# Attention and two MLP layers on one core: k and v in one buffer, constants in paired transfers, one row correction moved to GpSimd

## The reference, cut to what matters

```python
kv  = einsum('bhsd,bhse->bhde', k, v)          # linear attention
out = einsum('bhsd,bhde->bhse', q, kv)
x   = out / sqrt(mean(out*out, -1) + 1e-6) * g_norm
u   = x + real(fft(fft(x, axis=1), axis=2))    # over tokens, then over features
y   = u + relu(layer_norm(u) @ w_ch1) @ w_ch2  # first MLP
z   = y + (U, V mix of tokens)                 # rank 32
out = z + relu(z @ w2_ch1) @ w2_ch2            # second MLP
```

## Time and profile before

| what | value |
|---|---|
| median of the runs | 1747.55 us |
| the profiled execution | 1749.69 us |
| its span in the profile | 1747.9 us |
| mean granted TensorE clock | 0.995 of full |
| TensorE matmul busy | 1695.9 us (97%) |
| VectorE busy | 1377.2 us (79%) |
| GpSimd busy | 223.1 us (13%) |
| bytes moved by DMA | 478.15 MB, 274 GB/s in the mean |

### The profile page before, as it was taken

The page is one execution under the profiler, slowest core; times in us unless marked ns, Lnnn a source line. Parts: engine busy times, 40 slices in busy tenths (PEclk is TensorE's granted clock), DMA queues, the critical chain, the costliest instruction groups (busy, mean ns, idle before and its releaser), DMA issues.

```text
span 1747.9 us, 27408 instructions
## 1 busy us (share of the span) xinstructions
PE 1695.9 (97%) x10712; PEld 1643.6 (94%) x10712; DVE 1377.2 (79%) x1741; ACT 802.0 (46%) x1163; POOL 223.1 (13%) x170
## 2 busy tenths in 40 slices
PE   5999989899999999999999999999999999999999
PEld 5888779899999999999999999999999999999999
DVE  5999989988887987986976867957857758659567
ACT  2344646545445445445444445434434444343343
POOL 0464320020020020020110110100100100100200
PEclk9999999999999999999999999999999999999999
DMA  8785569998988898898986777966867767767663
GB/s 252 253 278 193 212 240 363 382 343 303 328 312 307 325 318 303 321 323 306 317 284 241 287 235 267 335 226 243 281 220 251 267 237 253 265 223 252 226 249 122
DMA packets 118753, 478.15 MB, mean 274 GB/s; under 512 B 12897, under 2 KB 40865, under 8 KB 77922
## 3 DMA queue, kind: packets, MB, share of 16 engines
q1 hardware_dynamic: 118258, 475.22, 77.1%
q10 hardware_dynamic: 368, 1.18, 0.2%
HBM read 396.14 MB, written 78.64 MB: 272 GB/s over the span
## 4 chain that ended last, share of the span: by engine, by line
PE 77%; DVE 16%; issue 4%; DMA 3%; ACT 1%; SPq 0%; DVEq 0%; ACTq 0%
PE pair L977 11%; PE pair L978 11%; PE pair L979 11%; PE pair L1008 6%; PE pair L1009 6%; PE pair L1010 6%; PE pair L997 5%; PE pair L1000 5%; PE pair L999 5%; DVE t_lo L1628 4%; DMA sseq_sb<-s_seq 2%; PE pair L750 2%; DVE t_raw L1647 2%; PE pair L771 2%; PE tr_ps L865 1%
## 5 line engine op out<-in xcount | busy, mean ns | idle before, releaser
L977 PE MATMUL pair<-t_hi,w_sb 128*128 128x384 f32 x1344 | 461.6, 343 | 9.1 <-DVE h_sb L1665 7.2
L978 PE MATMUL pair<-t_lo,w_sb 128*128 128x384 f32 x1344 | 456.1, 339 | 0.0
L979 PE MATMUL pair<-t_hi,w_sb 128*128 128x384 f32 x1344 | 455.8, 339 | 0.0
L1295 ACT ACTIVATE t_hi<-t_raw 128x768 fp32r<-128x768 f32 x240 | 203.1, 847 | 280.0 <-DVE t_raw L1647 279.9
L1628 DVE TENSOR_TENSOR t_lo<-t_raw,t_hi 128x768 fp32r<-128x768 f32 x300 | 303.1, 1016 | 16.0 <-ACT t_hi L1283 14.6
L1874 POOL TENSOR_TENSOR t_raw<-a_sb 128x768 f32<-128x768 f32 x60 | 135.7, 2265 | 1277.5 <-PE pair L1000 553.6
L997 PE MATMUL pair<-w_sb,t_hi 128*128 128x256 f32 x1008 | 285.5, 283 | 8.7 <-DVE t_lo L1628 7.8
L999 PE MATMUL pair<-w_sb,t_hi 128*128 128x256 f32 x1008 | 282.7, 280 | 0.0
L1000 PE MATMUL pair<-w_sb,t_lo 128*128 128x256 f32 x1008 | 282.6, 280 | 0.0
L977 PEld LDWEIGHTS pair<-t_hi,w_sb 128*128 128x128 f32 x1344 | 253.3, 188 | 17.3 <-issue 12.7
L978 PEld LDWEIGHTS pair<-t_lo,w_sb 128*128 128x128 f32 x1344 | 253.2, 188 | 2.6
(11 more groups left out here) (189 smaller groups left out, 2196.3 us busy)
## 6 DMA issues: line engine op xcount, KB each, us to landing
w_sb<-wc SPq DMA_DIRECT2D x263, 1024.0 KB, 5.6
wc<-w_sb SPq DMA_DIRECT2D x25, 1024.0 KB, 6.6
w_raw<-wr1a SPq DMA_DIRECT2D x24, 512.0 KB, 7.6
w_raw<-wr1b SPq DMA_DIRECT2D x24, 512.0 KB, 4.1
w_raw<-wr2a SPq DMA_DIRECT2D x10, 1024.0 KB, 8.1
wc<-pb_v SPq DMA_DIRECT2D x16, 640.0 KB, 6.8
q_sb<-q_t SPq DMA_DIRECT2D x8, 1152.0 KB, 9.1
u_dram<-x_sb SPq DMA_DIRECT2D x24, 384.0 KB, 4.7
```

Of the source, the lines that this page charges most:

```text
L977: nc.tensor.matmul(ps, w_hi, hi[:, x, :], start=(fresh and x == 0), stop=False, skip_group_check=True)
L978: nc.tensor.matmul(ps, w_hi, lo[:, x, :], start=False, stop=False, skip_group_check=True)
L979: last = nc.tensor.matmul(ps, w_lo, hi[:, x, :], start=False, stop=(x == 1), skip_group_check=True)
L1295: nc.scalar.activation(t_hi[r][:, :, :], t_raw[r][:, :, :], ACT.Copy).then_inc(hi_ready, 1)
```

## The change

1. k and v stand in one buffer `in_kv`, [128, 5, 2, 512], and in one host tensor, and so each batch's `load_kv` is two transfers (1024 + 1024 KB in one, 128 + 128 KB in one) in place of four. Batch 0 comes in five pieces, one for each group of rows t, and each has its own semaphore: t = 0, 2 and the rest on SP, t = 1 and 3 on ScalarE's queue.
2. `cseq_sb` and `sseq_sb` become halves of one tensor `cs_sb`, [97, 2, 3, 289], loaded by one transfer; the sine half is padded from 96 to 97 rows. `cft_sb` and `sft_sb` become halves of `cf_sb`, [128, 2, 2, 257], also one transfer.
3. `fix_row(6)` goes from VectorE to GpSimd, between `add_transform(6, 1)` and `raw(0, 0)`; `add_transform(6, 2)` goes behind `raw(0, 0)`.
4. `copy_cos` of ScalarE waits for `ds_ready` of the batch before in place of `u_added`, and for `row_fixed` at tile 0 alone.

```diff
-    cseq_sb = at("cseq_sb", a0 + 38944, [PT + 1, NT, KC])
-    sseq_sb = at("sseq_sb", a0 + 42432, [PT, NT, KC])
+    cs_sb = at("cs_sb", a0 + 38944, [PT + 1, 2, NT, KC])
+    cseq_sb, sseq_sb = cs_sb[:, 0, :, :], cs_sb[0:PT, 1, :, :]
...
-                sp.dma_start(flat(k_sb[r][:, 0:4, :]), flat(k_main[b])).then_inc(kv_loaded[r], 16)
-                sp.dma_start(k_sb[r][0:64, 4, :], k_rest[b]).then_inc(kv_loaded[r], 16)
-                sp.dma_start(flat(v_sb[r][:, 0:4, :]), flat(v_main[b])).then_inc(kv_loaded[r], 16)
-                sp.dma_start(v_sb[r][0:64, 4, :], v_rest[b]).then_inc(kv_loaded[r], 16)
+                sp.dma_start(in_kv[r][:, 0:4, :, :].rearrange("p t x n -> p (t x n)"),
+                             kv_main[b].rearrange("p t x n -> p (t x n)")).then_inc(kv_loaded[r], 16)
+                sp.dma_start(flat(in_kv[r][0:64, 4, :, :]), flat(kv_rest[b])).then_inc(kv_loaded[r], 16)
...
-            for t in range(2):
-                sp.dma_start(flat(k_sb[0][:, 2 * t:2 * t + 2, :]), flat(k_main[0][:, 2 * t:2 * t + 2, :])).then_inc(kv0_loaded[t], 16)
-            sp.dma_start(k_sb[0][0:64, 4, :], k_rest[0]).then_inc(kv0_loaded[2], 16)
+            for t in (0, 2):
+                sp.dma_start(flat(in_kv[0][:, t, :, :]), flat(kv_main[0][:, t, :, :])).then_inc(kv0_loaded[t], 16)
+            sp.dma_start(flat(in_kv[0][0:64, 4, :, :]), flat(kv_rest[0])).then_inc(kv0_loaded[4], 16)
...
-            sp.dma_start(flat(cseq_sb[:, :, :]), flat(c_seq)).then_inc(const_loaded, 16)
-            sp.dma_start(flat(sseq_sb[:, :, :]), flat(s_seq)).then_inc(const_loaded, 16)
+            sp.dma_start(cs_sb[:, :, :, :].rearrange("p x t n -> p (x t n)"),
+                         cs_seq.rearrange("p x t n -> p (x t n)")).then_inc(const_loaded, 16)
             load_kv(2)
-            sp.dma_start(flat(cft_sb[:, :, :]), flat(c_feat)).then_inc(feat_loaded, 16)
-            sp.dma_start(flat(sft_sb[:, :, :]), flat(s_feat)).then_inc(feat_loaded, 16)
+            sp.dma_start(cf_sb[:, :, :, :].rearrange("p x t n -> p (x t n)"),
+                         cs_feat.rearrange("p x t n -> p (x t n)")).then_inc(feat_loaded, 16)
...
                 if not first:
-                    act.wait_ge(u_added, NT * (b - 1) + t + 1)
-                    act.wait_ge(row_fixed, b)
+                    act.wait_ge(ds_ready, NT * (b - 1) + t + 1)
+                    if t == 0:
+                        act.wait_ge(row_fixed, b)
...
                     unfold(b - 1, 2, first)
                     sum_slot(1)
-                    fix_row(b - 1)
...
-                for t in range(NT):
+                for t in range(NT if b < B - 1 else 2):
                     add_transform(b - 1, t)
+            fix_row(B - 2)
             raw(0, 0)
+            add_transform(B - 2, 2)
             raw(0, 2)
             raw(0, 3)
```

More of the change, by code:

```diff
@@ L175, in in_load_at, with build_program @@
     return t, t + 2
-def build_program(nc, k_main, k_rest, v_main, v_rest, q_t, g_norm, wr1a, wr2a, wr1b, wr2b, u_perm, v_perm,
-                  c_seq, s_seq, c_feat, s_feat, eye, u_dram, x2_dram, wc1, wc2, out):
+def build_program(nc, kv_main, kv_rest, q_t, g_norm, wr1a, wr2a, wr1b, wr2b, u_perm, v_perm,
+                  cs_seq, cs_feat, eye, u_dram, x2_dram, wc1, wc2, out):
     F32 = mybir.dt.float32
@@ L195, in build_program @@
     sets = (base + 31744, base)
-    k_sb = [at(f"k_sb{r}", sets[r], [128, 5, D]) for r in range(2)]
-    v_sb = [at(f"v_sb{r}", sets[r] + 10240, [128, 5, D]) for r in range(2)]
+    in_kv = [at(f"in_kv{r}", sets[r], [128, 5, 2, D]) for r in range(2)]
     q_sb = [at(f"q_sb{r}", sets[r] + 20480, [128, NP, 2 * NT * PT]) for r in range(2)]
@@ L216, in build_program @@
     ds_sb = at("ds_sb", a0 + 57760, [PT, NT, 2, LC])
-    cft_sb = at("cft_sb", a0 + 63936, [128, 2, LC])
-    sft_sb = at("sft_sb", a0 + 66016, [128, 2, LC])
+    cf_sb = at("cf_sb", a0 + 63936, [128, 2, 2, LC])
+    cft_sb, sft_sb = cf_sb[:, 0, :, :], cf_sb[:, 1, :, :]
     gn_sb = at("gn_sb", a0 + 68096, [PT, HD])
@@ L347, in build_program @@
         gn_loaded = sem("gn_loaded")
-        kv0_loaded, q0_loaded = [sem(f"kv0_loaded{n}") for n in range(3)], sem("q0_loaded")
+        kv0_loaded, q0_loaded = [sem(f"kv0_loaded{n}") for n in range(5)], sem("q0_loaded")
         kv_loaded, q_loaded = [[sem(f"{what}_loaded_{r}") for r in range(2)] for what in ("kv", "q")]
@@ L737, in first_kv_products @@
                         cols = slice(128 * h, 128 * (h + 1))
-                        last = nc.tensor.matmul(kv_ps[:, cols], k_sb[0][0:rows, t, cols], v_sb[0][0:rows, t, cols],
+                        last = nc.tensor.matmul(kv_ps[:, cols], in_kv[0][0:rows, t, 0, cols], in_kv[0][0:rows, t, 1, cols],
                                                 start=(t == 0 and h == 0), stop=(t == 4), skip_group_check=True)
@@ L749, in kv_products @@
                         rows = 128 if t < 4 else 64
-                        last = nc.tensor.matmul(kv_ps[:, cols], k_sb[r][0:rows, t, cols], v_sb[r][0:rows, t, cols],
+                        last = nc.tensor.matmul(kv_ps[:, cols], in_kv[r][0:rows, t, 0, cols], in_kv[r][0:rows, t, 1, cols],
                                                 start=(t == 0), stop=(t == 4))
@@ L1226, in phase1_step @@
                         ln_total(q)
-            for t in range(2):
-                act.dma_start(flat(v_sb[0][:, 2 * t:2 * t + 2, :]), flat(v_main[0][:, 2 * t:2 * t + 2, :])).then_inc(kv0_loaded[t], 16)
-            act.dma_start(v_sb[0][0:64, 4, :], v_rest[0]).then_inc(kv0_loaded[2], 16)
+            for t in (1, 3):
+                act.dma_start(flat(in_kv[0][:, t, :, :]), flat(kv_main[0][:, t, :, :])).then_inc(kv0_loaded[t], 16)
             act.wait_ge(warm_zeroed, 1)
@@ L1845, in add_transform, with fix_row @@
                 last.then_inc(u_added, 1)
+            def fix_row(b):
+                pool.wait_ge(u_added, NT * b + 1)
+                pool.wait_ge(mrow_ready, b + 1)
+                mirr = x_sb[b % 3][0:1, 1, :]
+                nc.gpsimd.tensor_tensor(mirr[:, 0:LC], mrow_sb[:, b % 2, 0:LC], nyq_sb[:, :], ALU.add)
+                nc.gpsimd.tensor_tensor(mirr[:, LC:D], mrow_sb[:, b % 2, LC:D], nyq_sb[:, 255:0:-1],
+                                        ALU.add).then_inc(row_fixed, 1)
             def sum_unit(unit):
@@ L1922, in transform_constants @@
     s_feat = np.sin(2 * np.pi * (((i[:, None] + 1) * l) % D) / D)
-    both = [a.reshape(2, 128, LC).transpose(1, 0, 2) for a in (c_feat, s_feat)]
-    return [np.ascontiguousarray(a, dtype=np.float32) for a in (c_seq, np.sin(angle), *both)]
+    s_seq = np.zeros((PT + 1, NT, KC))
+    s_seq[:PT] = np.sin(angle)
+    feat = np.stack([c_feat, s_feat]).reshape(2, 2, 128, LC).transpose(2, 0, 1, 3)
+    return [np.ascontiguousarray(a, dtype=np.float32) for a in (np.stack([c_seq, s_seq], axis=1), feat)]
 def kernel(q, k, v, g_norm, moe_w_ch1, moe_w_ch2, moe2_U, moe2_V, moe2_w_ch1, moe2_w_ch2):
@@ L1949 @@
     q_t = np.asarray(q)[:, :, order, :].reshape(B, NP, 2, PT, 2 * NT, HD).transpose(0, 2, 5, 1, 4, 3)
-    (k_main, k_rest), (v_main, v_rest) = rows(k), rows(v)
-    c_seq, s_seq, c_feat, s_feat = transform_constants()
+    kv = np.stack([rows(k), rows(v)], axis=2)
+    cs_seq, cs_feat = transform_constants()
     ins = {
-        "k_main": k_main, "k_rest": k_rest, "v_main": v_main, "v_rest": v_rest,
+        "kv_main": kv[:, :512].reshape(B, 128, 4, 2, D), "kv_rest": kv[:, 512:],
         "q_t": q_t.reshape(B, 128, NP, 2 * NT * PT), "g_norm": np.asarray(g_norm),
```

13 lines of the change are left out of this document (6 added, 7 removed).

## The result

The changed kernel takes **1757.5 us** in the median of five runs (1755.56 to 1759.53), against 1747.55 for the kernel before, run beside it (five runs, 1745.23 to 1752.44). The ratio is 1.0055, with a 95% interval of 1.0043 to 1.0067: slower by 0.55%. The profiled execution took 1757.5 us, its span 1755.7 us, 7.8 more than the span before, at a mean granted clock of 0.989 (before 0.995).

A forecast was written before the change was run, and what follows sets the result against it. TensorE, busy 97% of the span, was taken as the bound, so only its waits count: constants +10.3, seam -4.9, sum +5.4 us on the median 1747.55, giving 1753.0 us; 8-in-10 range 1748 to 1761.

The forecast's parts named there:

- +10.3 predicted: At the start, the paired constants land 10.3 us later, near 54.2 us, and TensorE starts its first transform there.
- the 24.7 that I took over: Time in us from which the prediction had the 97 cosine rows going through one DMA engine in the kernel before.
- a longer idle time costs no more than a few tenths: TensorE's half clock after its wait for the constants: a few tenths of a us more at most, left out.
- The rival that the constants land no later: At the start, constants land before 45.3 us; seam and up to 0.7 us remain, 1742; chance 0.07 with other faster ways.
- Edit 1 at nothing: The k and v loads: any saving ends under the wait for the constants, so priced at nothing.
- worth up to about 0.7 us: Start, were the constants on time: the fold's end at 43.30 and VectorE's chain would decide, worth up to about 0.7 us.
- 4.9 predicted: Seam at 217 to 230 us: step 6 starts at 239.1 in place of about 244.0, a gain of 4.9 us.
- I count one GpSimd instruction of delay each time: At the seam, VectorE's two-input instructions each wait for one GpSimd instruction; `lo_up(0, 0)` ends near 221.4 us.
- The rival of the held VectorE: VectorE held behind GpSimd's whole run at the seam: it gives 1.9 us, 1756; inside the forecast's chance of 0.61.
- the row of 6.33 us at 217.00: Seam in the profile before: a wait at 217.00 spanning several GpSimd instructions, 6.33 us; used as the bound of 1.9.
- the row of 2.60: Profile before: VectorE's L1628, 0.9 us each at 236.75, took 2.60 us where its list meets GpSimd's `raw`.

The follow-up runs named there:

- 96 + 1 rows: The changed kernel with the token constants split by rows, one transfer of rows 0 to 95 and one of row 96: 1747.92 us, ratio 0.9995.
- 112 rows: The changed kernel with the sequence constants padded from 97 to 112 rows, still one transfer: 1748.61 us, ratio 0.9996.
- the hold: GpSimd waits before `raw(0, 2)` until VectorE has written weight slot 0's low part; added to the changed kernel with constants in two transfers: 1740.51 us, ratio 0.9953.
- the kernel of edits 3, 4 and the hold: The kernel before with edits 3 and 4 alone and GpSimd's wait ahead of `raw(0, 2)`: 1744.42 us, ratio 0.9976.
- both holds with 112 rows: The changed kernel with constants padded to 112 rows, GpSimd's first sums held until batch 0's fold is done, and its wait before `raw(0, 2)`: 1741.52 us, ratio 0.9951.
- two products thrown away: The changed kernel with constants in two transfers and GpSimd's seam wait, plus two unused TensorE products before the wait for the fold: 1740.63 us, ratio 0.9954.
- Fourteen products during the wait: The changed kernel with 14 more TensorE products, results thrown away, between batch 0's attention and the wait for the constants: 1754.48 us, ratio 1.0035.
- the kernel with two halves: The changed kernel with its token constants loaded by two transfers again, of 97 and 96 rows; the rest of the change stays: 1744.96 us, ratio 0.9984.

## Why the prediction was right, and where it was not

**The sign and the place were right.** The chain begins with `cs_sb`, TensorE stands 12.5 us (I had said 13), the DMA share is 0.07 at 27 GB/s, SP is held behind it, the batches are the old ones shifted by 10, and the seam gives back less than that. The measured 1757.5 lies in the range; the middle was 4.5 us too low.

**The constants: +10.3 predicted, +10.2 measured, by errors that cancel.** The duration on the engine was sized well. The trace's packets show the 97 rows of 6936 bytes on one engine from 21.24 to 51.67 us, 30.4 us (predicted 29.5), 0.265 us each when alone. The start was not: the rows begin 3.5 us earlier than the 24.7 that I took over, because edit 1 shortens what lies ahead. Edit 2 without edit 1 lands at 55.5, 1.3 us from the 54.2 predicted. And the clock was mis-sized: "a longer idle time costs no more than a few tenths" stands against 2.0 us in this trace. Of these 0.5 lie in the stretch behind the wait, much as said (9.55 us against 9.09), and 1.5 in L749 (7.61 against 6.06). A slow L749 came in four traces, after waits of 0, 1.09, 2.92 and 12.53 us, so its 1.5 us cannot be put down to the length of the wait, and that it closes the sum at +10.2 is luck. The rule of the Trainium skill on the divisor (page "DMA: Bandwidth & Descriptors", section "Why a DMA increments its semaphore by 16 and not by 1") agrees with the traces: one transfer of 97 wide rows took 30.4 us from its first row to its last, 96 + 1 rows 3.5 and 112 rows 4.0.

**The rival that the constants land no later** would have needed them before 45.3 us. It fell. What it said of the rest held in its direction and at half its size: with the constants on time the seam and the start win 2.8 us by ratio (1744.96) where it had 5.6 (1742).

**Edit 1 at nothing was wrong.** The step that failed is "worth up to about 0.7 us": I took the fold's end at 43.30 as given, but the fold hangs on batch 0's k and v. With them in five pieces the first product starts at 5.9 us in the changed kernel (7.0 before), and the fold ends at 42.0 in place of 43.30. In the eight traces with edit 1 and without GpSimd beside the fold it ends at 40.8 to 42.1, in the four without the edit at 41.7 to 43.7. Alone, the edit wins 3.1 us (ratio 0.9982, 0.9972 to 0.9991). Which part of the earlier fold comes from the pieces and which from the fewer issues was not tried apart.

**The seam: 4.9 predicted, 2.8 measured.** The step that failed is "I count one GpSimd instruction of delay each time". The rival of the held VectorE is what happened: 6.00 us, to the end of GpSimd's run of six instructions, `t_lo` ending at 236.6, which on the old clock (10.2 less) is 226.4 against the rival's 226.6. Its 1.9 was nearer than my 4.9. Two of my signs failed with it: TensorE stands 4.67 us where I had said no more than 3, and the first L977 comes 3.5 us earlier on the old clock, not 8. I had both before me, the row of 6.33 us at 217.00 and the row of 2.60, and went by the second; the first had it. The Trainium skill, page "SBUF — State Buffer", section "Who interferes with whom", has the later instruction wait until the first has finished; the runs show it waiting for a whole run of them. With the hold, what I had counted on comes about: `t_lo` is short, TensorE waits for `m2` before step 6, and step 6 starts at 238.9 on the old clock, where I had 239.1. So the seam then gives the 4.9 at the place where I had sized it, in all four traces; at the first read it is 3.9, because the sums for later entries come late in turn (ScalarE waits 3.74 us for GpSimd's next `t_raw` in the kernel of edits 3, 4 and the hold). Why the medians show so little of it in two of the three pairs stays open. A smaller slip: I priced the two row instructions at 0.81 us each, and the second took 1.82, beside VectorE's `sum_slot` (226.10 to 227.31), so `row_fixed` came at 227.9 and ScalarE did wait for it, 0.65 us. And the prediction gives two sizes for `m2`: the sum puts it at 238.1, 3.8 us earlier, the signs say some 5.

**Against the sum.** +10.2 - 2.8 = +7.4 us at the first read, +7.8 at the end of the profile, against +5.4 predicted. The medians differ by 9.95: the profiled execution of before was itself 2.1 us above its median, that of the changed kernel was at its median. So of the 4.5 us between the middle of the forecast and the result 2.4 are the sum's and 2.1 come from which execution was profiled. Between 749 and 1148 us of the traces the shifts change by some 3 us at most in either direction from kernel to kernel; what decides that stayed open.

**The best version** by its time is the changed kernel with the constants in two halves and GpSimd's wait at the seam: 1740.51 us, 0.47% below the kernel before. Its ratio of 0.9953 can't be told from the 0.9951 of both holds with 112 rows and the 0.9954 with two products thrown away.

## What to carry to other kernels

Before two transfers are made one, count the rows: a tensor of 97 partitions goes through one DMA engine at 25 to 27 GB/s, and with rows twice as wide the constants took 30.4 us from the first row to the last, in place of 18.7, while what is queued behind them is held; pad it or split off the odd row. When such a brake is taken away, look at what then starts early: here GpSimd's sums fell onto VectorE's fold and cost some 2 us in the traces, and one wait on the engine with time to spare brought them back. A two-input VectorE instruction that starts beside a run of GpSimd instructions can be held for all of it (6.00 us here for 0.96 us of work), and a forecast should carry that price as a bound at least. And before a slow or fast stretch is put down to the wait ahead of it, look at the clock on both sides of the wait, and at a second trace of the same program.

## What the runs showed of the hardware that I had not expected

- VectorE's `t_lo` (0.96 us of work) lasted 5.99 to 6.00 us in each of the seven traces in which it began in the second of six GpSimd instructions that followed one another without a gap, and 2.47 or 2.48 us in the four in which there were four of them; each time it ended 0.8 us after the run. In the fold, where GpSimd's instructions were 128x256, VectorE's lasted 0.83 to 1.21 us in place of 0.42 to 0.68, so there it did get in between. Why it does in one place and not in the other was not tried.
- The clock around a wait: in the eight traces in which TensorE had stood 1.24 us or more, the stretch up to L749 took 9.1 to 10.8 us (the granted clock 0.50 in part of it), in the six with 0 to 1.09 us 7.3 to 7.4. That is not the wait's doing alone. The fold sets when the products with the constants may start, so the wait is short where the sixteen products ahead of it ran long: in the four traces with 0.83 to 1.09 us and nothing thrown away these took 3.4 to 3.6 us, at a granted clock of 0.52 to 0.55, in place of 1.99 at 1.00. The slow stretch had come ahead of the wait. With two products thrown away the clock was 1.00 on both sides. A second stretch at half clock, in L749, came in four traces (7.61 to 9.16 us in place of 6.06), with no rule that I can read off. Fourteen products during the wait cured the first and not the second.
- The parts of the change add up within the noise, 1.0080 (edit 2) times 0.9982 (edit 1) times 0.9982 (seam), 1.0044 against 1.0055 (1.0043 to 1.0067), but two of them do not: edit 1 and the seam edits give 0.9982 each, and the kernel with two halves, which has both, 0.9984 (0.9975 to 0.9993) and not 0.9964. Its trace has the seam's 2.8 us and a start 2.9 us later than that of edit 1 with the same program up to there, so it is the start that varies; what decides it stayed open.
